# Attention and two mixtures of experts in one launch: hidden weights kept in fp32 row groups, ten weight places, counts on TensorE, sort tables with tokens innermost

## What is computed

```python
# 1. attention, B=8, H=8, S=512, Ns=32, D=64
scores = scale * x @ state.T            # softmax over the 32 state rows
xread  = softmax(scores) @ state
scores2 = scale * state @ x.T           # softmax over the 512 rows of x
sread  = softmax(scores2) @ x
x = concat([xread, sread])              # 8 * (512 + 32) = 4352 tokens of 512
# 2. soft mixture, 8 experts with 4 slots each, F=1024
logits = x @ phi                        # 4352 x 32
slot_input = softmax(logits, axis=tokens).T @ x          # 32 x 512
slot_out[e] = relu(slot_input[e] @ w1[e]) @ w2[e]
x = softmax(logits, axis=slots) @ slot_out               # 4352 x 512
# 3. one expert per token
e_idx  = argmax(x @ w_gate)             # 8 experts
gate   = max softmax prob * sigmoid((x @ w_output_gate)[e_idx])
out    = gate * (relu(x @ v1[e_idx]) @ v2[e_idx])
```

## Time and profile before

| | us |
|---|---|
| median of 3 runs | 509.6 |
| lowest to highest | 508.0 to 510.34 |
| the profiled execution, its time | 508.22 |
| its span, first to last instruction | 506.4 |
| TensorE matmuls busy | 456.5 (90%), 3624 records |
| TensorE weight loads busy | 256.5 (51%) |
| VectorE, ScalarE, GpSimd busy | 137.8, 143.5, 139.5 |
| output product (L918), busy | 249.2 |
| mean granted clock of TensorE | 0.957 of 2.4 GHz |

### The profile page before, as it was taken

One profiled execution on the slowest core, in us unless ns is written; L12 is line 12 of the kernel. 1 busy time (PEld: TensorE's weight loads), 2 busy tenths in 40 slices (PEclk: granted clock), 3 DMA queues, 4 the chain that ended last, 5 costly groups with the idle time before them and its releaser, 6 DMA issues.

```text
span 506.4 us, 10287 instructions
## 1 busy us (share of the span) xinstructions
PE 456.5 (90%) x3624; PEld 256.5 (51%) x3625; DVE 137.8 (27%) x279; ACT 143.5 (28%) x330; POOL 139.5 (28%) x207
## 2 busy tenths in 40 slices
PE   6888886799978948799999999999999999999991
PEld 5676755553416625645454545545454554545440
DVE  2699898720001893201010101001010100101000
ACT  3878654301001535312121212212121221212110
POOL 3333513074000113312323323232332323233110
PEclk9999899989786978999999999999999999999997
DMA  8899446659999889777772011010101101010110
GB/s 281 279 375 306 185 168 230 272 187 413 430 426 432 343 332 393 264 253 220 250 251 94 27 45 45 27 47 25 48 28 44 45 27 44 27 48 21 42 44 2
DMA packets 29539, 88.89 MB, mean 176 GB/s; under 512 B 6174, under 2 KB 15394, under 8 KB 26432
## 3 DMA queue, kind: packets, MB, share of 16 engines
q1 hardware_dynamic: 25552, 78.06, 41.3%
q0 software_dynamic: 3952, 10.33, 6.0%
HBM read 78.14 MB, written 10.59 MB: 175 GB/s over the span
## 4 chain that ended last, share of the span: by engine, by line
PE 72%; DMA 10%; DVE 7%; issue 3%; SPq 2%; ACT 2%; POOL 2%; POOLq 0%; DVEq 0%; ACTq 0%
PE bank L918 49%; DMA arena<-in_moe_w 7%; PE bank L907 3%; PE bank L906 3%; DMA arena<-in_x 3%; PE bank L773 3%; SPq L292 2%; PE bank L821 2%; PE bank L561 1%; PE bank L550 1%; PE bank L809 1%; PE bank L574 1%; PE bank L591 1%; DVE rmx L1133 1%; DVE rsum L1164 1%
## 5 line engine op out<-in xcount | busy, mean ns | idle before, releaser
L918 PE MATMUL bank<-arena,z 128*128 x560 | 249.2, 598 | 0.9 <-DVE z L1428 0.8
L918 PEld LDWEIGHTS bank<-arena,z 128*128 128x128 f32 x560 | 103.6, 190 | 122.1 <-issue 120.0
L1428 DVE TENSOR_SCALAR z<-bank 128x512 f32<-128x512 f32 x35 | 24.2, 692 | 250.9 <-PE bank L907 250.9
L1095 ACT ACTIVATE z<-bank,tile_gate 128x512 f32<-128x512 f32 x35 | 24.0, 687 | 227.8 <-PE bank L918 227.8
L480 POOL COPY rows_to<-sidx 128x1 int32 (+1 forms) x35 | 6.4, 181 | 152.5 <-ACT z L1095 152.5
L488 POOL DMA_INDIRECT z<-token_rows,rows_from x36 | 37.9, 1054 | 29.0 <-POOL rows_from L480 29.0
L498 POOL DMA_INDIRECT out<-z,rows_to x35 | 35.7, 1019 | 29.8 <-POOL rows_to L480 29.8
L906 PE MATMUL bank<-cT,parts 128*128 128x128 bf16 x280 | 36.4, 219 | 0.5 <-issue 0.5
L907 PE MATMUL bank<-cT,parts 128*128 128x128 bf16 x280 | 36.5, 219 | 0.1
L906 PEld LDWEIGHTS bank<-cT,parts 128*128 x280 | 27.4, 98 | 1.3 <-issue 0.9
L907 PEld LDWEIGHTS bank<-cT,parts 128*128 x280 | 27.4, 98 | 1.0 <-issue 0.5
(11 more groups left out here) (228 smaller groups left out, 506.9 us busy)
## 6 DMA issues: line engine op xcount, KB each, us to landing
arena<-in_moe_w SPq DMA_DIRECT2D x31, 2048.0 KB, 12.3
arena<-in_x SPq DMA_DIRECT2D x7, 1024.0 KB, 8.5
parts<-in_moe_w SPq DMA_DIRECT2D x1, 2048.0 KB, 8.9
token_rows<-z SPq DMA_DIRECT2D x8, 162.0 KB, 2.8
arena<-in_x SPq DMA_DIRECT2D x2, 512.0 KB, 5.4
z<-token_rows,rows_from POOLq DMA_INDIRECT x36, 2.6
out<-z,rows_to POOLq DMA_INDIRECT x35
z<-in_state SPq DMA_DIRECT2D x1, 512.0 KB, 3.6
```

The source lines that it names most:

```text
L918: mm = e.matmul(pY[p][:, :], hT[p][:, c, :], arena[:, bass.ds(ex * UNIT + 512 * c, 512)], start=(c == 0), stop=(c == CF - 1))
L1095: e.activation(ysb[p], pY[p][:, :], ACT.Copy, scale=tile_gate[:, q:q + 1])\
L1428: e.tensor_scalar(hT[p][:, 4:8, :], bank[2 * p + 1][:, :].rearrange("p (c t) -> p c t", c=4), 0.0, None, ALU.max).then_inc(relu_v, 1)
```

## The change

- **G stays fp32.** No parts, no spread, no `gA` and `gB`. ScalarE copies each G once from its bank to `gAll` (32 slots of four quarters, 256 columns each), and G products rotate over four banks. For each tile VectorE copies the expert's 256 columns to `gNow[p]`, two tiles ahead. The hidden product is eight fp32 matmuls in four row groups: K = 32, 128 columns of weights, 128 moving, group g into bank g.
- **c stays fp32.** A table row is 33 words. It is turned by four matmuls against the identity into four column groups of one bank, so that each row group has c.
- **Relu** is in four pieces of 256 columns, two on ScalarE and two on VectorE; the four banks are shared by all tiles, where there were two pairs.
- **Ten weight places**: the lower half of `parts` is the tenth, and `SLOT` is new. What lay there (`cT4`) moved to `z2`, the gathered rows too.
- **SP sends loads 8 to 23 in one loop.** The table goes out in three stores from ScalarE's queue, behind its copies of g0 and g1 and a wait for the gates.
- **Counts on TensorE**: `hot` in bf16, one matmul with the triangle and 34 with ones of shrinking width add up over groups in PSUM. The scan over 8 experts is one multiply with a triangle `upto` and one reduction.
- **Tables with tokens innermost**, all operands bf16; lane numbers are laid out beforehand by GpSimd (`lane_mat`, in the place of load 15, so v2[4] waits for the tables).
- **Sort behind the sixth product** (`SORT_AFTER = 5`). The row buffers are cleared before, and the first four gathers take their numbers from `sidx` itself.

The diff, cut to its core:

```diff
-SLOT = [0, 1, 2, 5, 6, 4, 7, 3] + [8, 0, 1, 2, 5, 6, 4, 7] + [3, 5, 6, 4, 7, 3, 5, 6]
+SLOT = [0, 1, 2, 5, 6, 4, 7, 3] + [8, 9, 0, 1, 2, 5, 6, 4] + [7, 3, 8, 0, 1, 2, 5, 6]
 NU = 3 * NE
+LANES = SLOT[2 * NE - 1]
...
-        gA = parts[:, 0:UNIT].bitcast(BF16)
-        gB = parts[:, UNIT:2 * UNIT].bitcast(BF16)
+        gAll = parts[:, 0:NE * GW]
+        gNow = [parts[:, NE * GW + GW * q:NE * GW + GW * (q + 1)] for q in range(2)]
...
-        lane_hot = z1[:, 0:NT * P // 2].bitcast(BF16).rearrange("p (t l) -> p t l", t=NT)
-        tile_hot = z1[:, NT * P // 2:NT * P // 2 + NT * ST // 2].bitcast(BF16).rearrange("p (t s) -> p t s", t=NT)
+        lane_hot = z1[:, 0:NT * P // 2].bitcast(BF16).rearrange("p (l t) -> p l t", t=NT)
+        tile_hot = z1[:, NT * P // 2:NT * P // 2 + NT * ST // 2].bitcast(BF16).rearrange("p (s t) -> p s t", t=NT)
...
-        pG = bank[4:6]
-        pC = bank[6][:, 0:P].bitcast(BF16)
+        pG = [bank[4], bank[5], bank[0], bank[1]]
+        pC = bank[6][:, 0:P]
...
-            for u in range(8, 21):
-                load_w(u)
-            e.wait_ge(row_ready, 2)
...
-            for u in range(21, NU):
+            for u in range(8, NU):
                 load_w(u)
             for ex in range(NE):
                 wait_used(e, max(v for v in range(NU) if SLOT[v] == ex))
+                if ex == LANES:
+                    e.wait_ge(lane_ready, 2)
...
+            e.tensor_copy(rowbuf[:, :, 0:NS], comb).then_inc(row_ready, 1)
...
-            def part_3(ex):
-                if ex >= 2:
-                    e.wait_ge(spread_psum, ex - 1)
-                e.wait_ge(g2_done, ex + 1)
-                e.tensor_tensor(gp[ex % 2][2], rG[ex % 2], gp[ex % 2][1], ALU.subtract).then_inc(g3_done, 1)
...
+            e.wait_ge(w_used, 2 * NE)
+            e.tensor_copy(lane_mat, lane[:, :].unsqueeze(2).to_broadcast([P, P, NT])).then_inc(lanes_laid, 1)
+            for q in range(4):
+                e.memset(row[q], 0.0).then_inc(row_zero, 1)
+            e.wait_ge(row_zero, 4)
             e.wait_ge(sidx_ready, 1)
-            e.wait_ge(sort_psum, 1)
-            e.memset(z1[:, 0:4 * ROWW], 0.0).then_inc(row_zero, 1)
-            e.wait_ge(row_zero, 1)
-            e.wait_ge(table_out, 16 * 2 * NB)
+            e.wait_ge(table_out, 16 * 3)
...
-                gather(t, t, first=True)
+                gather_row(t, sidx[:, t:t + 1])
...
-                if ex >= 2:
-                    e.wait_ge(gr_done, ex - 1)
+                if ex >= 4:
+                    e.wait_ge(g_kept, ex - 3)
                 w = slot(SLOT[u]).rearrange("p (c n) -> p c n", c=CD)
                 for c in range(CD):
                     for q in range(4):
-                        mm = e.matmul(pG[ex % 2][32 * q:32 * q + 32, 0:256], soT[:, c, 0:NS],
-                                      w[:, c, 256 * q:256 * q + 256], start=(c == 0), stop=(c == CD - 1))
+                        mm = e.matmul(pG[ex % 4][32 * q:32 * q + 32, 0:GW], soT[:, c, 0:NS],
+                                      w[:, c, GW * q:GW * q + GW], start=(c == 0), stop=(c == CD - 1))
                 mm.then_inc(g_psum, 1)
...
             def count_experts():
-                e.wait_ge(hot_ready, 1)
-                e.matmul(pT[:, 0:NT * NE], upper[:, :], hot, start=True, stop=True)
-                e.matmul(pL[:, 0:NT * NE], ones[:, :], hot, start=True, stop=True).then_inc(count_psum, 1)
+                e.wait_ge(hot_ready, 2)
+                e.matmul(pT[:, 0:NE * (NT + 1)], upper[:, :], hot_pad, start=True, stop=False, skip_group_check=True)
+                for t in range(NT):
+                    mm = e.matmul(pT[:, NE * (t + 1):NE * (NT + 1)], onesb[:, :],
+                                  hot_bf[:, t, :].unsqueeze(1).to_broadcast([P, NT - t, NE]), start=False,
+                                  stop=(t == NT - 1), skip_group_check=True)
+                mm.then_inc(count_psum, 1)
             def sort_rows():
-                e.wait_ge(lane_ready, 4)
+                e.wait_ge(lane_ready, 3)
                 for t in range(NT):
-                    mm = e.matmul(pT[:, 0:2 * ST], lane_hot[:, t, :], tile_id[:, t, :, :], start=(t == 0),
+                    mm = e.matmul(pT[:, 0:2 * ST], lane_hot[:, :, t], tile_id[:, :, :, t], start=(t == 0),
                                   stop=(t == NT - 1))
                 mm.then_inc(sort_psum, 1)
-            hidden_weights(0)
-            hidden_weights(1)
-            count_experts()
-            e.wait_ge(pick_ready, 4)
             e.wait_ge(l2_copied, 2)
-            spread(0)
-            for ex in range(2, NE):
-                if ex == NE - 2:
+            for ex in range(NE):
+                hidden_weights(ex)
+                if ex == 1:
+                    count_experts()
+                if ex == SORT_AFTER:
                     sort_rows()
-                hidden_weights(ex)
-                spread(ex - 1)
-            spread(NE - 1)
...
             e.wait_ge(sidx_ready, 1)
...
             keep_clock(16, pL)
-            e.wait_ge(ga_ready, 2 * NE)
-            e.wait_ge(gb_ready, 2 * NE)
+            e.wait_ge(g_kept, NE)
...
-                e.transpose(pC[:, 0:P], row_bf[q][:, 0:P], identb[:, :])
-                e.transpose(pC[:, P:2 * P], row_bf[q][:, NS:NS + P], identb[:, :]).then_inc(c_psum, 1)
+                for g in range(4):
+                    mm = e.matmul(pC[NS * g:NS * g + NS, :], row[q][:, 0:NS], ident[:, :], start=True, stop=True)
+                mm.then_inc(c_psum, 1)
             def hidden(t, p, wait=True):
-                ex = expert(t)
                 e.wait_ge(c_copied, t + 1)
+                e.wait_ge(g_copied, t + 1)
                 if wait:
-                    e.wait_ge(relu_a, t - 1)
-                    e.wait_ge(relu_v, t - 1)
-                for c in range(CF):
-                    dst = bank[2 * p + c // 4][:, P * (c % 4):P * (c % 4) + P]
-                    e.matmul(dst, gA[:, bass.ds(ex * F + P * c, P)], cT[p][:, 0:P], start=True, stop=False)
-                    mm = e.matmul(dst, gB[:, bass.ds(ex * F + P * c, P)], cT[p][:, P:2 * P], start=False, stop=True)
+                    e.wait_ge(relu_a, 2 * t)
+                    e.wait_ge(relu_v, 2 * t)
+                for h in range(2):
+                    for g in range(4):
+                        mm = e.matmul(bank[g][:, P * h:P * h + P], gNow[p][32 * g:32 * g + 32, P * h:P * h + P],
+                                      cT[p][32 * g:32 * g + 32, :], start=True, stop=True)
                 mm.then_inc(hid_psum, 1)
             def output(t, p, wait=True):
                 ex = expert(t)
                 e.wait_ge(v2_ready, ex + 1)
-                e.wait_ge(relu_a, t + 1)
-                e.wait_ge(relu_v, t + 1)
+                e.wait_ge(relu_a, 2 * t + 2)
+                e.wait_ge(relu_v, 2 * t + 2)
...
-            def part_1(ex):
+            def keep_g(ex):
                 e.wait_ge(g_psum, ex + 1)
-                e.activation(gp[ex % 2][0], pG[ex % 2][:, 0:256], ACT.Copy).then_inc(g1_done, 1)
...
+                e.activation(gAll[:, GW * ex:GW * ex + GW], pG[ex % 4][:, 0:GW], ACT.Copy).then_inc(g_kept, 1)
...
             e.activation(el, t8, ACT.Exp).then_inc(gexp_done, 1)
-            part_1(0)
-            part_2(0)
-            part_1(1)
+            keep_g(0)
             e.wait_ge(egate_ready, 1)
             e.activation(st1[:, :], st1[:, :], ACT.Exp, scale=-1.0).then_inc(eexp_done, 1)
-            part_2(1)
+            keep_g(1)
+            e.wait_ge(row_ready, 2)
+            by_batch = table.rearrange("(b r) w -> b r w", b=NB)
+            for f in range(2):
+                e.dma_start(by_batch[4 * f:4 * f + 4, S:S + NS, :], rowbuf[:, NB * J + f, :]).then_inc(table_out, 16)
+            e.dma_start(by_batch[:, 0:S, :].rearrange("b (p j) w -> p b (j w)", j=J),
+                        rowbuf[:, 0:NB * J, :].rearrange("p (b j) w -> p b (j w)", b=NB)).then_inc(table_out, 16)
             for ex in range(2, NE):
-                spread_out(ex - 2)
-                part_1(ex)
-                part_2(ex)
-            spread_out(NE - 2)
-            spread_out(NE - 1)
+                keep_g(ex)
...
-                e.activation(hT[p][:, 0:4, :], bank[2 * p][:, :].rearrange("p (c t) -> p c t", c=4), ACT.Relu)\
-                 .then_inc(relu_a, 1)
+                for g in range(2):
+                    e.activation(hT[p][:, 2 * g:2 * g + 2, :], bank[g][:, 0:GW].rearrange("p (c t) -> p c t", c=2),
+                                 ACT.Relu).then_inc(relu_a, 1)
...
-            n = 11
-            e.wait_ge(count_psum, 1)
...
-            e.tensor_tensor(t8, pT[:, 0:NT * NE].rearrange("p (t e) -> p t e", t=NT), pre[cur], ALU.add)\
+            e.tensor_scalar(cnti[:, :], cnti[:, :], 7, 7, ALU.logical_shift_right, ALU.logical_shift_left)\
              .then_inc(route, 1)
...
-            e.tensor_tensor(t8, t8, tstart[:, :].unsqueeze(1).to_broadcast([P, NT, NE]), ALU.add).then_inc(route, 1)
```

(39 more changed lines are left out.)

287 lines of the change are left out of this document (91 added, 196 removed).

## The result

The changed kernel takes **518.85 us** (median of 4 runs, 517.12 to 520.96); the kernel before took 509.44 beside it (4 runs, 508.0 to 510.34). The ratio is 1.0189, 95% interval 1.0141 to 1.0237: slower by 9.4 us, where 494 was forecast. The profiled execution took 520.96 us, its span is 519.2, 12.8 longer than before's 506.4.

What follows compares the result with a forecast made beforehand. TensorE alone was taken to bound the kernel from 215.5 us, with two weight transfers in the chain before. 508.2 - 20 (earlier start) + 6 (longer tiles) = 494.2, said as 494; range 484 to 507.

Steps and rivals of the forecast that it cites:

- Step 2: Table stores move from SP to ScalarE's queue, three instead of sixteen; load 21 leaves earlier, load 23 lands at 185.5.
- third rival: Weight transfers: table stores and v2 share engines with weights, or half clock slows w2; 10 us lost, 504; chance 0.11.
- signs of being wrong: Tiles over 8.6 us apart with hidden passes over 0.05 apart; or first output product after 200, released by v2[0] or a gather.
- Step 5: Tile loop: turning c, fp32 hidden product and tiling changes take 1.17 us, 0.17 more a tile, 6 us more in 35.
- changes of tiling: TensorE's three switches of tile shape in each tile of the loop: 0.49 us together.
- Step 1: Weight loads: with ten places, loads from 9 on land 4.9 us earlier; w2 ends at 147.3 instead of 152.2.
- Step 4: Start of the tiles: without split and spread, the first output product comes at 195.5, bounds 191.2 and 199.
- lower bound of 191.2: Earliest start of the first output product, set by the arrival of v2[0].
- Step 3: Routing and sort: counting 2.2 us, tables 9.8 (no change), sort 6.1 from its weight load's step, gathers start at 188.3.
- Loads bare: Hidden product: each pass waits for its own weights, a tile 0.59 us longer than now; 509, no change; chance 0.12.
- row groups take turns: Hidden product: fp32 loads of different groups go one after another, 1.46 us more a tile; 539, slower; chance 0.09.
- Transfers don't move up as far: Weight transfers: shared engines or half clock in the w2 stage lose 10 of the 20 us gained; 504; chance 0.11.

Runs made afterwards that it cites:

- e1: The changed kernel with TensorE's read of the tile's expert number moved to the head of the step: 502.89 us, ratio to the kernel before 0.9828.
- e6: The changed kernel with e1's edit and the table laid out by partition, stored in one transfer, output rows worked out on VectorE: 491.90 us.
- n1: e6 with nine weight places again, in the order of the kernel before: 495.84 us, ratio to the kernel before 0.9758.
- e7: The changed kernel with e1's edit and the lane table laid out with lanes innermost, so the sort's stationary operand is dense: 504.73 us (one run).
- e9: e6 with the sort's moving operand made dense and the sort put behind the fifth product: 494.18 us, ratio to the kernel before 0.9714.
- e10: e6 with the hidden product's passes reordered so that the two halves of one row group follow one another: 495.36 us (one run).

## Why the prediction was wrong

**Step 2 failed: the store's own landing was left out of the sum.** The prediction priced what the stores free on SP and said that the copies behind them cost nothing. It gave the gathers' start by the sort alone (188.3) and no time for the store to land among full weight traffic. That is a failure to count the moved step's transfer on the queues that it now runs beside: before, SP's order put the loads behind the store. It took 27.85 us, where before the stores had landed in 2.8, and cost 502.89 - 491.90 = 11.0 us by the medians of e1 and e6. Counted from the U product it is 111.2 - 100.3 = 10.9 with these two profiles, and 108.1 - 100.25 = 7.9 with the changed kernel's. The third rival, with a chance of 0.11, named the shared engines and the size (10 us), but as weights that come late. The weights came in time (the last v1 product ends at 191.1 in e6, forecast 189.9); the store was late. One of the prediction's own signs of being wrong, a first output product later than 200 behind a gather, came: 211.03, with TensorE idle for 7.23 us until the first gather had landed.

**Step 5 failed: it priced passes and left the register read out.** With the read in its place the gap is 0.53 us a tile (e1: 1.55 to 1.02), 16.0 us. In the kernel before it had cost 0.15, unseen inside the 1.00 us. Of the sign of being wrong one half came (tiles 8.61 us apart) and the other didn't: the passes lie 41 ns apart, under the 0.05 us that were named. Opposite to it, the changes of tiling were oversized: 0.49 in three, where 1.02 us in all hold eight turning passes and sixteen hidden ones (these alone 16 x 0.041 = 0.66, forecast 0.45); the sum of 1.17 was 0.15 too long, 5 us.

**Together:** 494.2 + 16.0 + 11.0 - 5.3 = 515.9 us, a rough sum, as its terms are medians of different groups of runs. The profiled execution can be added up by stage. Its span of 519.2 is 26.8 above the forecast 506.4 - 20 + 6 = 492.4. The first output product is 211.03 - 195.5 = 15.5 late: 5.5 by the attention phase, 7.9 by the store, and 2.1 that e6 has too (197.62). The tiles take 308.2 - (290.9 + 6) = 11.3 more: 17.4 by the read (e6 takes 290.8), less 6.1 by which the passes were oversized.

**What was right.** Step 1: 4.9 us at the end of w2 forecast, 152.4 against 147.5 measured (n1 and e6), and the forecast end was 147.3. Step 4: with both faults mended the first output product is at 197.62, forecast 195.5, and the last v1 product ends at 191.1, forecast 189.9. But its lower bound of 191.2 was that of v2[0] (191.6 in e6), and the first tile waits for v2[1], 197.3. And that e6 comes so near to 494, with 491.90, is in part luck: a start 2.1 us too late and tiles 6.1 us shorter than forecast partly cancel. Step 3's count: 2.2 us forecast, 2.28 measured.

**Right in sum, wrong inside.** The sort: 6.1 us forecast from the weight load's step, 5.2 measured, but e7 and e9 show that it is the moving operand. VectorE's tables: "no change, 9.8 us" was the bound I took; they took less:

```profile
175.15 0.88 DVE L1273 TENSOR_TENSOR z<-arena,dtile 128x1394 bf16<-128x1394 bf16 x1
175.95 2.42 DVE L1276 TENSOR_TENSOR z<-arena,dlane 128x4352 bf16<-128x4352 bf16 x1
178.28 1.60 DVE L1280 TENSOR_TENSOR z<-z,idb 128x2788 bf16<-128x2788 bf16 x1
```

4.9 us against 5.04 + 3.12 and 1.60 for the tile table, 9.8, before. The Trainium skill ("VectorE: DVE Perf Modes", what auto-detection actually checks) gives two elements a cycle to an operation whose tensors are all of 16 bits and of step one. By that rule the new form takes half the time, and the rows agree. It gained nothing here, as the sort stood behind product 5 anyway (tables ready at 179.9, the sort at 183.20).

**The rivals.** *Loads bare* and *row groups take turns* fall: 16 passes in 0.66 us, and the order doesn't matter (e10). *Transfers don't move up as far* was right that the start gains less, by another transfer than it named, and has no part in the loop. No rival had the loop slower by anything but TensorE's passes, and so the sign was missed.

## What to carry to other kernels

Cost every wait that a change puts on the path by the landing of its transfer, among the traffic that will then be there: a store in 1304 pieces beside full weight traffic took 27.85 us, in 144 pieces 11.2, and in 1304 pieces with the weights held back 6.31. Put reads of registers at the head of a step, where the engine still has work queued: the same read cost 0.53 us a tile behind short matmuls, 0.15 behind the matmuls of the kernel before, and nothing measurable at the head. When two limits lie behind each other, mend both before judging a part: ten places were worth 3.9 us beside them, and the changed kernel's edits with these two mended take 491.90 us against 509.6.
